# A fused attention and two-layer expert kernel: a second row buffer, other places for casts and splits at chunk edges, and another row order, one scatter loop and nested turns in the last layer

## The reference

```python
# u, v: (4, 2496, 256)   z: (4, 2496, 64)
scores = (1.0 / S) * z @ z.transpose(0, 2, 1)
x = (u * (np.maximum(scores, 0.0) ** 2 @ v)).reshape(9984, 256)

# layer 1: 8 experts of 256 -> 1024 -> 256, only rows with x @ w_skip > 0
e = argmax(x @ w_gate); p = softmax(x @ w_gate)[e]
x[rows] = x + p * (relu(x @ w1[e]) @ w2[e])

# layer 2: the same weights, other gate and a bias per modality
e = argmax(x @ w_gate2 + bias[modality]); p = softmax(...)[e]
out = p * (relu(x @ w1[e]) @ w2[e])
```

## Time and profile before

| what | value |
|---|---|
| median of 3 runs | 1515.71 us |
| the profiled execution | 1515.54 us |
| its span | 1514.0 us |
| mean granted TensorE clock | 0.993 |
| attention, 0 to 720 us: TensorE busy | 702.39 of 720.00 us |
| first layer, 739 to 1027 us: TensorE busy | 287.87 of 288.00 us |
| second layer, 1031 to 1495 us: TensorE busy | 462.22 of 464.00 us |
| 1495 to 1514 us: TensorE busy | 0.00 of 19.00 us |

### The profile page before, as it was taken

One profiled execution on the slowest core, in us unless ns is written; L12 is line 12 of the kernel. 1 busy time (PEld: TensorE's weight loads), 2 busy tenths in 40 slices (PEclk: granted clock), 3 DMA queues, 4 the chain that ended last, 5 costly groups with the idle time before them and its releaser, 6 DMA issues.

```text
span 1514.0 us, 34658 instructions
## 1 busy us (share of the span) xinstructions
PE 1468.2 (97%) x11861; PEld 1292.1 (85%) x11861; DVE 1011.9 (67%) x2377; ACT 773.6 (51%) x1544; POOL 401.1 (26%) x379
## 2 busy tenths in 40 slices
PE   8999999999999999999899999999999999999994
PEld 7888978789888888788799999998888888888884
DVE  7989977999789998987666666665333333333331
ACT  6676767776677767665344444444333332333331
POOL 4133312334123424212322222224121221221211
PEclk9999999999999999999999999999999999999997
DMA  5311030212202020201533354323211111111110
GB/s 119 98 33 62 28 99 28 65 42 62 79 31 65 28 86 28 85 30 36 170 109 130 129 201 131 104 95 109 73 43 43 44 69 41 42 54 46 42 50 21
DMA packets 58018, 107.86 MB, mean 71 GB/s; under 512 B 18007, under 2 KB 32354, under 8 KB 57884
## 3 DMA queue, kind: packets, MB, share of 16 engines
q0 software_dynamic: 18464, 58.68, 11.1%
q1 hardware_dynamic: 39420, 47.48, 11.1%
HBM read 75.63 MB, written 32.04 MB: 71 GB/s over the span
## 4 chain that ended last, share of the span: by engine, by line
PE 81%; DVE 5%; issue 5%; DMA 4%; ACT 1%; POOL 1%; SPq 0%; POOLq 0%; ACTq 0%; DVEq 0%
PE pO L1436 23%; PE pS L1684 11%; PE pO L1696 10%; PE pS L1644 9%; PE pO L1627 9%; PE pS L1425 6%; PE pO L1698 5%; PE pM L1684 3%; DVE AH L1091 3%; DMA raw<-in_v_dram 2%; DMA token_rows<-xrow,dest 1%; PE pT L1675 1%; PE pT L1574 1%; PE pO L1445 1%; POOL token_rows L527 1%
## 5 line engine op out<-in xcount | busy, mean ns | idle before, releaser
L1093 DVE TENSOR_TENSOR AL<-A,AH 128x512 fp32r<-128x512 f32 (+1 forms) x400 | 314.4, 786 | 13.7
L1436 PE MATMUL pO<-AH,VH 64*128 64x512 f32 (+1 forms) x1520 | 306.7, 384 | 9.2 <-DVE xT L998 7.2
L1436 PE MATMUL pO<-AL,VH 64*128 64x512 f32 (+1 forms) x1520 | 305.4, 382 | 0.0
L1436 PE MATMUL pO<-AH,VL 64*128 64x512 f32 (+1 forms) x1520 | 305.1, 382 | 0.0
L709 ACT ACTIVATE R<-pS 128x512 f32<-128x512 f32 (+1 forms) x400 | 213.5, 588 | 150.4 <-PE pS L1425 134.8
L1091 DVE CAST AH<-A 128x512 fp32r<-128x512 f32 (+1 forms) x400 | 231.7, 579 | 39.8 <-ACT A L718 39.4
L718 ACT ACTIVATE A<-R 128x512 f32<-128x512 f32 (+1 forms) x400 | 229.8, 624 | 19.8 <-DVE AL L1093 19.4
L1696 PE MATMUL pO<-VL,AH 128*128 128x512 f32 x640 | 232.4, 399 | 0.0
L1351 DVE SCALAR_TENSOR_TENSOR AL<-pS,AH 128x512 fp32r<-128x512 f32 x120 | 83.0, 692 | 180.8 <-ACT AH L877 179.3
L1436 PEld LDWEIGHTS pO<-AH,VH 64*128 64x128 f32 x1520 | 154.2, 184 | 34.4 <-issue 12.6
L1698 PE MATMUL pO<-VL,AL 128*128 128x256 f32 x640 | 179.5, 280 | 0.0
(11 more groups left out here) (241 smaller groups left out, 2477.5 us busy)
## 6 DMA issues: line engine op xcount, KB each, us to landing
raw<-in_w_dram POOLq DMA_DIRECT2D x22, 1024.0 KB
A<-token_rows SPq DMA_DIRECT2D x21, 536.0 KB
uT<-in_u_dram SPq DMA_DIRECT2D x16, 512.0 KB
xin<-token_rows SPq DMA_DIRECT2D x24, 268.0 KB
raw<-in_v_dram SPq DMA_DIRECT2D x4, 1152.0 KB, 5.8
A<-in_w2t_dram POOLq DMA_DIRECT2D x8, 512.0 KB
raw<-in_v_dram SPq DMA_DIRECT2D x4, 768.0 KB, 8.1
raw<-in_z_dram SPq DMA_DIRECT2D x8, 368.0 KB
```

The lines of the kernel that those rows point to most:

```text
L1093: v_.tensor_tensor(AL[k % NBUF][:, 0:n], A[k % NA][:, 0:n], AH[k % NBUF][:, 0:n].bitcast(F32), ALU.subtract).then_inc(al_ready, 1)
L1436: last = t_.matmul(pO[:, (KD * r + d) * QW:(KD * r + d) * QW + n], vv[rows, vo + k * D + d * P:vo + k * D + (d + 1) * P], a[k % NBUF][rows ...
```

## The change

**Two row buffers.** `chunk_rows` holds `xrow` and `xkeep` (a buffer of the second half of the kernel, free until then); a chunk uses the one of its parity, and `rows_stored` becomes two semaphores. ACT, and DVE in `row_meta`, wait for the scatter two chunks back. The table `dest` of row addresses stays single, and DVE gets a wait for the scatter of the previous chunk before it writes it.

**Places of casts and splits.** ACT's V and Z casts move from steps 1, 3, 5, 7, 9 to steps 3, 4, 5, 6, 8. The fifth Z part is cast, and its low part made, in the first chunk of the next batch. `xrow_half(g, 0)` moves from step 6 to step 7. The split of the first weights is spread over chunks 16 and 17.

**Last chunk.** Its logits come before its transposes, which take 128 rows at a time, and three waits go.

**Second layer.** layer1(7) stands before layer2(4), and `layer2_last` sums f = 5, 6, 7 for one group of rows after the other. POOL gets one loop over all tiles for its scatters. The loads of later weights move to SP and their low parts to DVE. On ACT, DVE and TensorE the turns are nested: the next turn is entered only if tiles are left.

```diff
+MIDDLE = (3, 4, 5, 6, 8)
+SPLIT_AT = ((B - 1) * QC + 1, (B - 1) * QC + 2)
...
+        chunk_rows = [xrow, xkeep[:, :, :, :].rearrange("p b s d -> p (b s) d")]
...
+        def stored_rows(idx):
+
+            return rows_stored[idx % 2], (STORED if idx % 2 else 0) + 64 * ((idx + 1) // 2)
...
+                    def load_weights_behind(turn_):
+
+                        sp.wait_ge(wl_ready, WP * turn_ + 2 * WP)
+                        sp.sem_inc(sp_passed, 1)
+                        e = sp.value_load(order[0:1, turn_ + 2:turn_ + 3], min_val=0, max_val=2 * E - 1)
+                        sp.dma_start(stage1, w1[ds(e, 1), :, :].rearrange("o (k p) f -> p (o k) f", p=P)).then_inc(w1_loaded, 16)
+                        sp.dma_start(stage2, w2[ds(e, 1), :, :].rearrange("o (f p) d -> p (o f) d", p=P)).then_inc(w2_loaded, 16)
...
-                for n, (raw, wh, wl) in enumerate(weight_pieces(0)):
+                for m, p in enumerate((4, 7)):
+                    n = 2 * (g - SPLIT_AT[0]) + m
+                    raw, wh, wl = weight_pieces(0)[n]
                     wait(wh_ready, n + 1)
                     for half in range(2):
-                        wait(al_ready, 2 + KT * g + 2 * (2 * n + half + 2))
+                        wait(al_ready, 2 + KT * g + 2 * (p + half + 1))
                         w = half_piece(n, half)
...
-                    g_.indirect_dma_start(xs, bass.IndirectOffsetOnAxis(dest[:, j:j + 1], 0), xrow[:, j, :], None,
-                                          bounds_check=GR * CAP - 1, oob_is_err=False).then_inc(rows_stored, 16)
+                    g_.indirect_dma_start(xs, bass.IndirectOffsetOnAxis(dest[:, j:j + 1], 0), chunk_rows[idx % 2][:, j, :], None,
+                                          bounds_check=GR * CAP - 1, oob_is_err=False).then_inc(rows_stored[idx % 2], 16)
...
+                if c == 0 and b > 0:
+                    z_low(b, NG - 1)
...
-                        for n in range(NG):
+                        for n in range(NG - 1):
                             z_low(b + 1, n)
-                if g == (B - 1) * QC + 1:
+                if g in SPLIT_AT:
                     split_low_first(g)
+                if g == SPLIT_AT[1]:
                     pool.wait_ge(wl_ready, WP)
                     load_weights(1)
...
-            for ph in range(2):
...
-                            if ph == 1:
-                                scatter_out(t)
...
+            next_weights(E, 0, True)
+            scatter_out(0)
+            pool.wait_ge(cum_ready, 2)
+            total = pool.value_load(cum[0:1, 1, E:E + 1], min_val=0, max_val=64)
+            with pool.If(total > 1):
+                with pool.Fori(1, total) as t:
+                    scatter_out(t)
...
+                if idx > 1:
+                    act.wait_ge(*stored_rows(idx - 2))
+                if idx == CHUNKS:
+                    s_.copy(chunk_rows[idx % 2][:, 2 * half:2 * half + 2, 0:D], pT[:, :].rearrange("p (t d) -> p t d", d=D)).then_inc(xrow_copied, 1)
+                    return
                 if half == 0:
                     act.wait_ge(lcols_made, idx)
-                    if idx == CHUNKS:
-                        act.wait_ge(route_step, ROUTE * idx + 1)
-                elif idx < CHUNKS:
+                else:
                     act.wait_ge(prefix_ready, idx)
-                act.wait_ge(rows_stored, 64 * idx)
-                to = xrow[:, 2 * half:2 * half + 2, 0:D].rearrange("p t (k r c) -> p r t k c", k=KD, r=2)
...
+                    if p == 7 and g > 0:
+                        xrow_half(g, 0)
...
-                    if p % 2 == 1 and b < B - 1:
+                    if p in MIDDLE and b < B - 1:
+                        m = MIDDLE.index(p)
                         if c == QC - 3:
-                            if p == 1:
+                            if m == 0:
                                 act.wait_ge(pv_done, KT * QC * b + NBUF)
-                            v_high(b + 1, p // 2)
+                            v_high(b + 1, m)
                         elif c == QC - 2:
-                            v_high(b + 1, VU // 2 + p // 2)
-                        elif c == QC - 1:
-                            z_high(b + 1, p // 2)
-                    if g == (B - 1) * QC + 1 and p % 2 == 1 and p // 2 < WP:
-                        if p == 1:
+                            v_high(b + 1, VU // 2 + m)
+                        elif c == QC - 1 and p != 6:
+                            z_high(b + 1, min(m, NG - 2))
+                    if p == MIDDLE[0] and c == 0 and b > 0:
+                        z_high(b, NG - 1)
+                    if g in SPLIT_AT and p in (3, 6):
+                        if g == SPLIT_AT[0] and p == 3:
                             act.wait_ge(pv_done, KT * QC * (B - 1) + NBUF)
-                        split_high(0, 0, p // 2)
-                    if p == 6 and g > 0:
-                        xrow_half(g, 0)
+                        split_high(0, 0, 2 * (g - SPLIT_AT[0]) + (p == 6))
...
-                lo = 1
-                for at in range(E):
+                def turns(at, lo):
+
...
+                    if at + 1 < E:
+                        with act.If(hi < total):
+                            turns(at + 1, hi)
+
+                turns(0, 1)
...
+                if idx > 1:
+                    dve.wait_ge(*stored_rows(idx - 1))
                 v_.tensor_tensor(dest[:, :], dest_f[:, :], invalid[:, ds(4 * idx, 4)], ALU.add).then_inc(dest_ready, 1)
...
+                    def weights_ahead():
+
+                        with dve.If(hi < total):
+                            next_low(at + E + 1, 1 - at % 2)
...
+                            if at > 0:
+                                with dve.If(t == lo):
+                                    weights_ahead()
...
+                    if at + 1 < E:
+                        with dve.If(hi < total):
+                            turns(at + 1, hi)
+
+                turns(0, 1)
...
+                        if idx == CHUNKS:
+                            last = t_.transpose(pT[:, (2 * i + kd) * P:(2 * i + kd + 1) * P], xT[:, kd, (2 * half + i) * P:(2 * half + i + 1) * P], ident[:, :])
+                            continue
...
+                def row_sums(h, f, s):
+
+                    rows = slice(s * P, (s + 1) * P)
+                    t_.matmul(pO[:, s * QW:(s + 1) * QW].rearrange("p (m d) -> p m d", m=2), AH[f][:, rows], w2hl[h][:, :, f, 0:D],
+                              start=(f == 0), stop=(f == NF - 1), skip_group_check=True)
+                    return t_.matmul(pO[:, s * QW:s * QW + D], AL[f][:, rows], w2h[h][:, f, 0:D],
+                                     start=False, stop=(f == NF - 1), skip_group_check=True)
+
...
-                        if f == NF - 1:
-                            last.then_inc(q.y_made, 1)
-                    if f < NF - 1:
-                        last.then_inc(q.h_used, 1)
+                        last = row_sums(h, f, s)
+                    last.then_inc(q.h_used, 1)
+
+                def layer2_last(t, h, between=None):
+
+                    for s in range(SUB2):
+                        for f in range(NF - 3, NF):
+                            if s == 0:
+                                pe.wait_ge(q.h_split, NF * t + NF + f + 1)
+                            last = row_sums(h, f, s)
+                            if s == SUB2 - 1 and f < NF - 1:
+                                last.then_inc(q.h_used, 1)
+                        last.then_inc(q.y_made, 1)
+                        if s == 1 and between is not None:
+                            between()
...
-                for f in range(3, NF):
+                for f in range(3, NF - 1):
                     layer2(0, 0, f - 3)
                     layer1(0, 0, 0, f, hring_lead)
+                layer1(0, 0, 0, NF - 1, hring_lead)
+                layer2(0, 0, 4)
                 pe.wait_ge(q.h_split, NF + 6)
                 transpose_half(1, 0, pT)
-                layer2(0, 0, 5)
-                layer2(0, 0, 6)
-                transpose_half(1, 1, pT)
-                layer2(0, 0, 7)
+                layer2_last(0, 0, lambda: transpose_half(1, 1, pT))
                 pe.wait_ge(cum_ready, 2)
-                lo = 1
...
+                            layer1(t, par, h, 7, hring)
                             layer2(t, h, 4)
-                            layer1(t, par, h, 7, hring)
-                            layer2(t, h, 5)
-                            layer2(t, h, 6)
-                            layer2(t, h, 7)
-                    lo = hi
...
+                    if at + 1 < E:
+                        with pe.If(hi < total):
+                            turns(at + 1, hi)
+
+                turns(0, 1)
```

More of the change, by code:

```diff
@@ new lines, in scatter_rows @@
+            def scatter_rows(t):
+                wait(PH[0].dest, t)
+                for s_ in range(SUB):
```

(9 more changed lines are left out.)

120 lines of the change are left out of this document (53 added, 67 removed).

## The result

The changed kernel takes 1490.05 us, median of four runs (1489.09 to 1490.74), against 1515.82 of the kernel before in the same comparison: a ratio of 0.9831, 95% interval 0.9814 to 0.9848, 25.8 us. Of the two profiled executions the span falls from 1514.0 to 1487.2, by 26.8. One execution of one experiment (e6) ran at a mean granted clock of 0.751 and took 1803.41 us; it is left out, and e6's median is that of the other three.

What follows compares the result with a forecast made beforehand. With TensorE busy 97% of the span, only its idle stretches could give time. Terms 2.9 + 2.9 + 3.3 + 3.0 + 0.7 + 5.8 = 18.6 us off 1515.54 gave a forecast of 1497 us, range 1491 to 1505.

Steps and rivals of the forecast that it cites:

- V load: Attention, three windows: ACT's wait for the V load goes with the new cast steps, 3 x 0.98 = 2.9 us.
- Second row buffer: Attention: ACT's copy waits for the scatter two chunks back, saving TensorE 2.2 + 0.7 = 2.9 us.
- Batch edges: Attention, three edges: moving the fifth Z part's POOL subtraction behind the edge gives 3.3 us, bounds 0 and 4.5.
- rival 1: Attention: DVE is what is full, so edges and split give nothing and the time is 1503.2; chance 0.20.
- First weight split: Attention: eight POOL subtractions in one chunk become four in each of two, giving 3.0 us, bounds 0 and 3.8.
- The end: After the last matmul: earlier scatters and no walk of empty turns give 5.8 us, bounds 2.1 and 8.1.
- Passage: Between attention and the first layer: TensorE waits for the first rows' load anyway, so nothing is gained.
- Second layer, first tiles: Second MoE layer's start: an earlier half transpose removes or shortens TensorE's waits, 0.7 us together.
- First layer and loop: First MoE layer and second layer's loop of tiles: no TensorE idle row of weight, no cost, zero change.
- (2): Program end: the drain's end is tied to the last scatter, so the end gives 2.1, time 1500.6; chance 0.18.
- (3): Second layer's second turn: DVE's jumps over the weight block delay tiles, about 1516.4 or 1541 us; chance 0.05.
- (4): Edges don't depend on these waits and the end is fixed by something else: within 3 us; chance 0.05.

Runs made afterwards that it cites:

- e6: Changed kernel with the old order of the second layer's sums and the lead tile's transposes in their old places: 1491.59 us, median of three runs.
- e4: Changed kernel with the V casts on steps 1, 3, 5, 7, 9 again: 1493.64 us.
- e12: Changed kernel with one row buffer, row copy at step 6, V and Z casts on odd steps, fifth Z part before the edge, first weights split in one chunk: 1508.79 us.
- e11: Changed kernel with all five Z casts on odd steps and all five subtractions ahead of the batch edge: 1494.13 us.
- e1: Changed kernel with one row buffer again, the copy of rows staying at step 7: 1489.77 us.
- e9: Changed kernel with ACT's copy of rows at step 6 again, two row buffers kept: 1489.96 us.
- e2: Changed kernel with the cast and the subtraction of the fifth Z part back in front of the batch edge: 1493.22 us.
- e3: Changed kernel with only ACT's cast of the fifth Z part back before the batch edge, GpSimd's subtraction staying behind it: 1490.25 us.
- e10: Changed kernel with one row buffer and the copy of rows at step 6: 1499.12 us.
- e7: Changed kernel with TensorE walking all eight turns again, empty ones too: 1496.44 us.
- e8: Changed kernel with GpSimd's loop of scatters walking all turns, empty ones too: 1492.84 us.

## Why the prediction was wrong

The direction was right, and so were the waits that it named; two parts of the sum were too small, attention (12.1 for 17.1) and the end (5.8 for 8.2). The step that failed is the pricing of the stalls, in three ways: stretched chunks were measured against 35.20 us and by one window of three, where the undisturbed chunk of their kind takes 34.9 (V load); the row buffer's wait was priced by idle rows instead of whole windows; and a jump of 2.3 us was kept behind GpSimd's loop. One mechanism was incomplete: the second buffer was taken for the only cure of the copy's wait.

- **V load**, 2.9: cause right (e4), but the undisturbed chunk of that kind is 34.9 and not 35.20, and half a microsecond runs over into the fifth chunks. It is 4.0. The 36.18 us on which the term rests is one window; the other two of before are 36.26 and 36.43.
- **Second row buffer**, 2.9 from idle rows of 1.11, 1.11 and 0.72 us. Undoing it together with the copy's later step gave 4.9 (e12 over e11), since an idle row leaves out how much longer the chunk gets: the last one was 1.2 too long (31.13 for 29.96) for a row of 0.72. And the gain is not the buffer's alone: without it, the copy's move from step 6 to 7, which I did not price at all, does as much (e1, but for 0.5 us in one window), and without that move the buffer does (e9). I said that DVE's new wait for the single table costs nothing; no window shows a cost.
- **Batch edges**, 3.3: right in cause and size (3.3 in e2, none in e3). What I missed is that this term and the one before it are not two: in the chunks behind two edges one scatter's landing sets when the copy starts, however early the edge is, and the 2.2 us of these two would not have been gained without a cure for the copy (e10 against e12). The change has both, so the sum stood. The Trainium skill's rule of the shared port pair (SBUF — State Buffer, section Who interferes with whom) agrees with the cast's 1.48 us in e2; the conclusion that I drew from it for rival 1, that moving the work within a chunk gives nothing, does not: e3 and the changed kernel gain all of it.
- **First weight split**, 3.0: 3.8, the upper bound. The 0.8 that I left for the pair beside the routing did not come.
- **The end**, 5.8: 2.1 from the order as forecast (e6), and the walk as a bound, but I kept one jump of 2.3 us behind GpSimd's loop. There is none: the branch out of the loop is at 1478.23 and the drain at 1478.31, so the drain begins before the last scatter is issued and lasts 8.66 us. I had named a drain of another length as a sign of being wrong; this is what it pointed at. The term's other bound, 8.1, had no jump, and it is what came: 8.2. The nested turns on TensorE were necessary, as said (e7).
- **Passage**, 0: 0.6 less, 20.45 us for 21.02, which may be chance: the experiments with two buffers, whose passage is the same, take 19.1 to 20.6. The idle rows fell (0.34 and 4.60 us, where 2.93 and 3.21 stood), but TensorE worked longer at the lower clock, 5.50 us, where it was 3.40 before:

```profile
714.90:720.40 5.50, 5.50 (x59) 4.70 (x60) 3.24 (x16) 1.67 (x5) 1.95 (x2) 0.50 0.36 114
```

- **Second layer, first tiles**, 0.7: 1.7, not to be told from chance (e6).
- **First layer and loop**, 0: right; no idle TensorE row inside a tile of the loop.

Rivals: DVE is not what is full (1): with DVE busy 32.44 of 35.20 and 33.14 of 34.93 us TensorE never waits. The drain is not tied to the last scatter alone (2), as e8 shows. DVE's jumps (3) cost nothing that TensorE sees. That the edges hang on something else and the end is fixed (4) is out by e2 and by e6 to e8. The low end of the range added 2.3 for the jump, 1.7 for the clock and 2.0 for edges and split to the forecast gain, but nothing for the base of the windows or for the idle rows, where 3.1 of the missing 5.0 us in attention lay (V load 1.1, row buffer 2.0). No run undoes the last chunk's new order of logits and transposes, or the moved weight loads, by itself.

## What to carry to other kernels

Price a stall by the length of the whole window against an undisturbed window of the same kind, not by the idle row in front of one instruction. Before adding up two waits of one stretch, ask whether they end at the same event; if they do, taking one away only lengthens the other. Where a change brings two cures for one wait, undo each alone and both together, or the gain goes to the wrong one.

## What the runs showed that I had not expected

- A stop of 2.54 us in one piece left TensorE at a granted clock of 0.56 over the next 3.90 us and cost 4.4 us in all (e10), and one of 1.78 us was followed by 0.51 over 3.50 us; 2.59 us in two pieces, in e12, left the clock at 1.00.
- GpSimd's drain at the end takes 6.8 us, counted from the end of its last scatter's issue or from the end of its walk, whichever is later, in the changed kernel, e6, e8 and the kernel before.
- An empty turn costs TensorE a branch of 2.57 us at the median (e7); GpSimd's branch takes 45 ns, and six empty turns together kept it 2.8 us (e8). The Trainium skill, in Advanced Engine Details and Errata, section Control Flow Timing, gives about 108 ns; the measurement decides.
